# Attention transposes moved one step behind the scores, softmax sums sent through DRAM, and the ninth block put into the second half's PSUM bank

## The reference

```python
q_pool = q.reshape(B, H, S // 2, 2, D).mean(axis=3)          # S 1152, D 64: 576 queries a head
scores = scale * np.matmul(q_pool, k.transpose(0, 1, 3, 2))  # 576 x 1152 a head
scores = scores - np.max(scores, axis=-1, keepdims=True)
attn = np.exp(scores)
attn = attn / (np.sum(attn, axis=-1, keepdims=True) + 1e-09)
x = np.matmul(attn, v)          # -> 2304 tokens x 512
h = x @ w_in                    # 512 x 2048
g = np.maximum(h, 0.0) + alpha * np.minimum(h, 0.0)
return g @ w_out                # 2048 x 512
```

## Time and profile before

| | us |
|---|---|
| time, median of 3 runs (930.55 to 931.39) | 931.33 |
| the profiled execution, its own time | 932.26 |
| its span | 929.7 |
| PE busy in the span | 887.3 |
| DVE busy | 516.9 |
| ACT busy | 423.4 |
| POOL busy | 213.3 |

### The profile page before, as it was taken

The page is one execution under the profiler, slowest core; times in us unless marked ns, Lnnn a source line. Parts: engine busy times, 40 slices in busy tenths (PEclk is TensorE's granted clock), DMA queues, the critical chain, the costliest instruction groups (busy, mean ns, idle before and its releaser), DMA issues. The chain is left out here.

```text
span 929.7 us, 20770 instructions
## 1 busy us (share of the span) xinstructions
PE 887.3 (95%) x6896; PEld 623.2 (67%) x6896; DVE 516.9 (56%) x836; ACT 423.4 (46%) x963; POOL 213.3 (23%) x182
## 2 busy tenths in 40 slices
PE   3799999999999999999999999999999999999997
PEld 1455555555555555555545799989999999989995
DVE  2676767677767776767676344344444444343442
ACT  2566666666666666666666222222322222322222
POOL 2112111211121112111200323323232323323230
PEclk9999999999999999999999999999999999999999
DMA  7435423542354235523520122212422222322211
GB/s 186 106 83 135 119 65 82 133 121 63 82 133 123 60 82 133 127 57 82 133 71 1 59 68 58 67 62 63 136 57 68 57 68 61 132 59 66 65 36 68
DMA packets 36366, 79.57 MB, mean 86 GB/s; under 512 B 5360, under 2 KB 9456, under 8 KB 36336
## 3 DMA queue, kind: packets, MB, share of 16 engines
q1 hardware_dynamic: 33936, 74.48, 31.0%
q10 hardware_dynamic: 2400, 4.72, 1.5%
HBM read 74.46 MB, written 4.72 MB: 85 GB/s over the span
## 5 line engine op out<-in xcount | busy, mean ns | idle before, releaser
L432 DVE TENSOR_REDUCE neg_max<-s_ps 128x1 f32<-128x1152 f32 x144 | 194.1, 1348 | 16.6 <-DVEq L431 16.6
L573 PE MATMUL pv_ps<-pt,v_f 128*64 128x256 f32 (+1 forms) x1152 | 169.0, 414 | 0.0
L532 PE MATMUL s_ps<-k_f,q_f 64*128 64x512 f32 (+1 forms) x640 | 160.2, 626 | 5.2 <-PEq L543 5.2
L348 ACT ACTIVATE e_sb<-s_ps,neg_max 128x1024 f32<-128x1024 f32 x144 | 160.1, 1112 | 0.0
L587 PEld LDWEIGHTS slot_ps<-ident,e_sb 64*128 64x128 f32 x2304 | 86.0, 139 | 82.4 <-issue 82.4
L465 DVE COPY pt<-slot_ps 128x512 f32<-128x512 f32 x144 | 99.6, 692 | 61.3 <-DVEq L464 59.4
L341 ACT ACTIVATE e_sb<-s_ps,neg_max 128x128 f32<-128x128 f32 x144 | 52.9, 367 | 171.5 <-ACTq L340 171.5
L617 PE MATMUL slot_ps<-x_hi,wi_hi 128*128 128x384 f32 x384 | 129.5, 337 | 1.1 <-PEq L613 1.1
L617 PE MATMUL slot_ps<-x_lo,wi_hi 128*128 128x384 f32 x384 | 129.5, 337 | 0.0
L617 PE MATMUL slot_ps<-x_hi,wi_lo 128*128 128x384 f32 x384 | 129.0, 336 | 0.0
L479 DVE TENSOR_SCALAR e_sb<-slot_ps,alpha_sb 128x384 f32<-128x384 f32 x96 | 59.3, 618 | 123.2 <-DVEq L477 123.2
(11 more groups left out here) (46 smaller groups left out, 1098.8 us busy)
## 6 DMA issues: line engine op xcount, KB each, us to landing
q_raw<-in_q SPq DMA_DIRECT2D x64, 288.0 KB, 4.5
k_f<-in_k SPq DMA_DIRECT2D x64, 288.0 KB, 4.2
wi_raw<-in_w_in SPq DMA_DIRECT2D x48, 256.0 KB, 2.6
wo_raw<-in_w_out SPq DMA_DIRECT2D x48, 256.0 KB, 2.6
v_f<-in_v SPq DMA_DIRECT2D x32, 288.0 KB, 3.0
out<-pt ACTq DMA_DIRECT2D x6, 768.0 KB, 4.4
k_end<-in_k SPq DMA_DIRECT2D x64, 32.0 KB, 4.0
alpha_sb<-in_alpha SPq DMA_DIRECT2D x1, 8.0 KB, 4.7
```

Of the source, the lines that this page charges most:

```text
L348: nc.scalar.activation(e_sb[:, b * NKEY + at:b * NKEY + at + n], s_ps[:, S_AT[b] + at:S_AT[b] + at + n], ACT.Exp, bias=neg_max[:, b:b + 1] ...
L432: nc.vector.tensor_reduce(out=neg_max[:, b:b + 1], in_=s_ps[:, S_AT[b]:S_AT[b] + NKEY], op=ALU.max, axis=AX_X, negate=True).then_inc(max_r ...
L532: ins = nc.tensor.matmul(s_ps[to:to + m, S_AT[b] + at:S_AT[b] + at + BANK], q_f[2 * g + h][rows, first:first + m], k_f[2 * g + h][rows, at ...
L573: ins = nc.tensor.matmul(pv_ps[h * D:(h + 1) * D, 0:n], v_f[2 * g + h][:, a, :], pt[:, a, at:at + n], start=(a == 0), stop=(a == KT - 1))
```

## The change

1. **Lag.** In step `s`, PE now transposes tile `s - 1`. `e_sb` has three buffers instead of two. The wait for `exponential` of `s` moves from ahead of the transposes to ahead of `big_scores`. Everything that follows the transposes moves one step later (`PRODUCT`, `INVERT`, `SCALE`), and there is one more step at the end, which makes no scores.
2. **The ninth block.** It goes into the first 128 columns of `slot_ps[1]`, the bank that DVE empties. PE therefore waits for DVE's copy of that bank (`half1_copied`) ahead of the ninth transpose, and DVE waits for `ninth_ready` ahead of its copy of it. The score bank is no longer touched by it, and `bank2_ready` now tells of the small scores alone.
3. **Sums through DRAM.** `spread_inverse` and the ACT copy go. SP stores `inv_sum` (128 rows of 5 or of 4 values, transposed on the way) to a DRAM scratch `sums`, waits until that has landed, and loads it back twice, spread over 64 partitions each, into `inv_bc`. The store and the loads stand in SP's order between the other loads; the loads of `v` go behind them.
4. **Split of x.** `scale` writes the whole of `x` in fp32 (`x_f`). The two halves of pass 0 are split on POOL in the last steps of attention (`x_split`), those of passes 1 and 2 at the end of the pass before, by ACT (`x_high`, 1536 columns) and DVE (`x_low`, 1536 columns), and PE waits for `x_ready` ahead of the first `hidden_unit` of each half. The split parts of x, the weights and g lie in one tensor `ff`.

The core of the diff:

```diff
-    PRODUCT = {5: (0, (0, 1)), 6: (0, (2, 3)), 7: (0, (4, 5)), 8: (0, (6, 7, 8)),
-               0: (1, (0, 1)), 1: (1, (2, 3)), 2: (1, (4, 5)), 3: (1, (6, 7)), 4: (1, (8,))}
-    SPREAD = {6: 0, 1: 1}
-    INVERT = {4: 0, 8: 1}
-    FIRST = 6
+    PRODUCT = {6: (0, (0, 1)), 7: (0, (2, 3)), 8: (0, (4, 5)), 0: (0, (6, 7, 8)),
+               1: (1, (0, 1)), 2: (1, (2, 3)), 3: (1, (4, 5)), 4: (1, (6, 7)), 5: (1, (8,))}
+    INVERT = {5: 0, 0: 1}
+    SCALE = {1: 0, 6: 1}
+    FIRST = 7
...
-        NINTH = s_ps[:, 2 * BANK + P:2 * BANK + 2 * P]
+        NINTH = slot_ps[1][:, 0:P]
...
+            def store_sums(group):
+                a, b = GROUP_TILES[group]
+                sp.wait_ge(inv_ready, 1).then_inc(inv_ready, -1)
+                sp.dma_start(sums[a * P:b * P].rearrange("(t p) -> p t", p=P), inv_sum[:, a:b],
+                             allow_slow_non_contiguous=True).then_inc(inv_stored, 16)
+            def spread_sums(group):
+                _, _, n, first = GROUPS[group]
+                sp.wait_ge(inv_stored, 16).then_inc(inv_stored, -16)
+                for h in range(2):
+                    row = sums[GROUPS[group][h]:GROUPS[group][h] + n]
+                    sp.dma_start(inv_bc[h * D:(h + 1) * D, first:first + n],
+                                 row.rearrange("(o n) -> o n", o=1).to_broadcast([D, n])).then_inc(inv_bc_in[group], 16)
+            def sums_and_qk(pair, g):
+                store_sums(0)
+                load_q(pair * 2)
+                spread_sums(0)
+                sp.wait_ge(k_free[g], 1).then_inc(k_free[g], -1)
+                load_k(pair * 2, 2 * g), load_k(pair * 2 + 1, 2 * g + 1)
+                store_sums(1)
+                load_q(pair * 2 + 1)
+                spread_sums(1)
...
 PE, step:
-                pe.wait_ge(exp_done, 1).then_inc(exp_done, -1)
-                for i in range(2):
-                    pe.wait_ge(slot_free[i], 1).then_inc(slot_free[i], -1)
-                for a in range(2 * CH):
-                    at = s % 2 * NKEY + a * P
+                if s > 0:
                     for i in range(2):
+                        pe.wait_ge(slot_free[i], 1).then_inc(slot_free[i], -1)
+                    for a in range(2 * CH):
+                        at = (s - 1) % 3 * NKEY + a * P
...
+                if left >= 0:
+                    pe.wait_ge(exp_done, 1).then_inc(exp_done, -1)
                 if left > 1:
                     begin_scores(s + 2)
                     for ins in big_scores(s + 2):
                         ins.then_inc(s_ready, 1)
-                pe.wait_ge(ninth_free, 1).then_inc(ninth_free, -1)
+                if s > 0:
+                    pe.wait_ge(half1_copied, 1).then_inc(half1_copied, -1)
+                    transposed(s - 1, 2 * CH, NINTH).then_inc(ninth_ready, 1)
                 if left > 0:
                     pe.wait_ge(exp_cut_done, 1).then_inc(exp_cut_done, -1)
-                ins = transposed(s, 2 * CH, NINTH)
                 if left > 1:
-                    ins = small_scores(s + 2)
-                ins.then_inc(bank2_ready, 1)
+                    small_scores(s + 2).then_inc(bank2_ready, 1)
...
 DVE, step:
+                if t in SCALE and pair is not None:
+                    scale(SCALE[t], pair + (0 if s < 2 * TILES else 1))
+                    if SCALE[t] == 1:
+                        dve.sem_inc(v_free[1 - g], 1)
+                if s > 0:
+                    dve.wait_ge(tr_ready[1], 1).then_inc(tr_ready[1], -1)
+                    nc.vector.tensor_copy(pt_half((s - 1) % TILES, 1),
+                                          half_columns(slot_ps[1][:, :])).then_inc(half1_copied, 1)
...
+                if s > 0:
+                    dve.wait_ge(ninth_ready, 1).then_inc(ninth_ready, -1)
+                    nc.vector.tensor_copy(pt_ninth((s - 1) % TILES), NINTH).then_inc(slot_free[1], 1)
                 if left > 1:
+                    dve.wait_ge(bank2_ready, 1).then_inc(bank2_ready, -1)
                     row_max(s + 2)
```

More of the change, by code:

```diff
@@ L13, with build @@
 BANK = 512
-def build(nc, q, k, v, w_in, w_out, alpha, out):
+def build(nc, q, k, v, w_in, w_out, alpha, sums, out):
     HEADS, D, NKEY = k.shape
@@ L135, in build @@
         bank2_ready = sem("bank2_ready")
-        ninth_free = sem("ninth_free")
+        half1_copied = sem("half1_copied")
+        ninth_ready = sem("ninth_ready")
         slot_free = [sem(f"slot{i}_free") for i in range(2)]
         inv_ready = sem("inv_ready")
-        spread_ready = sem("spread_ready")
-        inv_bc_ready = sem("inv_bc_ready")
+        inv_stored = sem("inv_stored")
+        inv_bc_in = [sem(f"inv_bc{i}_in") for i in range(2)]
         pv_done = sem("pv_done")
         pv_free = sem("pv_free")
-        x_sb_free = sem("x_sb_free")
+        x_done = sem("x_done")
         x_hi_done = sem("x_hi_done")
@@ L178, in over_steps, with x_chunk, x_part @@
                     step(s, two * 2)
-            for s in range(FIRST, REST):
+            for s in range(FIRST, REST + 1):
                 step(s, 2 * BODIES, REST - 1 - s)
+        def x_chunk(n, h):
+            at = (2 * n + h) * TOK
+            return x_f[:, :].rearrange("p (d c) -> p d c", d=DT)[:, :, at:at + TOK]
+        def x_part(part, h):
+            return part[h].rearrange("p (d c) -> p d c", d=DT)
         def pt_half(t, half):
-            at = PT_AT[t] if half == 0 else PT_MIX if t == MIX else PT_AT[t] + HALF
+            at = PT_AT[t] + half * HALF
             return pt[:, 0:2 * CH, at:at + HALF]
@@ L403, in hidden @@
                     act.wait_ge(g_ready, 1).then_inc(g_ready, -1)
-                    nc.scalar.activation(g_hi[0][:, :], g_sb, ACT.Copy).then_inc(g_hi_done, 1)
+                    nc.scalar.activation(g_hi[0], g_sb, ACT.Copy).then_inc(g_hi_done, 1)
+                    if last and not last_pass:
+                        x_high(n + 1, 0)
                     if first:
@@ L414, in hidden @@
                     act.wait_ge(g_ready, 1).then_inc(g_ready, -1)
-                    nc.scalar.activation(g_hi[1][:, :], g_sb, ACT.Copy).then_inc(g_hi_done, 1)
+                    nc.scalar.activation(g_hi[1], g_sb, ACT.Copy).then_inc(g_hi_done, 1)
+                    if last and not last_pass:
+                        x_high(n + 1, 1)
                     if not (last_pass and isinstance(f, int) and f >= FT - 2):
@@ L443, in scale @@
                 dve.sem_inc(pv_free, 1)
-            def x_high(pair):
-                nc.vector.tensor_copy(x_hi[:, bass.ds(pair * NQ, NQ)], x_sb[:, :]).then_inc(x_hi_done, 1)
+                if group == 1:
+                    dve.sem_inc(x_done, 1)
             def invert(group):
@@ L501, in _, with x_low @@
             dve.wait_ge(alpha_in, 16).then_inc(alpha_in, -16)
[L502 to L503 removed]
+            scale(0, NPAIR - 1)
             for n in range(PASSES):
+                last_pass = n == PASSES - 1
+                def x_low(h):
+                    dve.wait_ge(x_hi_done, 1).then_inc(x_hi_done, -1)
+                    nc.vector.tensor_tensor(x_part(x_lo, h), x_chunk(n + 1, h), x_part(x_hi, h).bitcast(F32),
+                                            ALU.subtract).then_inc(x_ready, 1)
                 def hidden(f, i, first, last):
@@ L507, in hidden @@
                     if n == 0 and not first:
-                        scale(1)
-                        x_high(NPAIR - 1)
+                        scale(1, NPAIR - 1)
+                    if last and not last_pass:
+                        x_low(0)
                     unit(f, 1)
+                    if last and not last_pass:
+                        x_low(1)
                 over_hidden(dve, hidden)
@@ L545, in transposed @@
             def transposed(s, a, to):
[L546 removed]
+                at = s % 3 * NKEY + a * P
                 return nc.tensor.transpose(to, e_sb[:, at:at + P], ident[:, :])
[L549 to L562 removed]
             def product(group, g, tiles):
@@ L650, in _ @@
             over_steps(pe, step)
-            pe.wait_ge(x_ready, NPAIR - 2)
-            hidden_unit(0, 0, 0, 0)
+            hidden_unit(0, 0, 0, 0, 0)
             pe.wait_ge(slot_free[1], 1)
-            pe.wait_ge(ninth_free, 1).then_inc(ninth_free, -1)
-            product(1, 1, (0, 1))
-            spread_inverse(1, tail_ps)
-            product(1, 1, range(2, KT))
+            product(1, 1, range(KT))
             for n in range(PASSES):
```

201 lines of the change are left out of this document (83 added, 118 removed).

## The result

The changed kernel takes **969.89 us** (median of 4 runs, 966.65 to 971.02) against 931.12 (930.55 to 931.39) for the kernel before, timed beside it: a ratio of 1.041, 95% interval 1.039 to 1.044. The forecast was 936 with a range of 926 to 947. The sign was right and the size was not, by 34 us. The profiled execution is the quickest of the four, 966.65 with a span of 964.9 us.

The account below looks back on a forecast made before the run. PE was taken as the bound, its waits as what counts. Pairs + 2.1, start and end - 0.3, pass ends + 3.4, network start - 0.3 make + 4.9 on 932.26: 937.1, median 936.2, said as 936; range 926 to 947.

Parts of the forecast that it names:

- 15 pairs, undisturbed: Attention's 15 regular pairs: 31.05 us each against 30.91 before, + 2.1 us in all.
- start and end of attention: First steps and last steps of attention: together 32.3 us against 32.6 before, - 0.3 us.
- network: Splits of x at pass ends cost + 3.4 us; 8 spread matmuls fewer at the network's start give - 0.3.
- SP's queue: Store and load of the sums on SP take about 9 us, hidden with 8 us to spare.
- the sums come late: Rival: the sums' trip exceeds 17 us, each us beyond costing one in each pair; over 952 us, chance 0.06.
- the sum of a pair: One attention pair on PE: ninths 16.64, products 10.04 and smaller terms give 31.1 us, kept as 31.05, against 30.91.
- waits in a row: Rival: the small scores' own wait behind the ninth's adds 0.1 us in nine steps a pair; 941 to 952, chance 0.14.
- The whole new wait: PE's wait for DVE's copy ahead of the ninth transpose: ninths sum to 16.64 against 14.04, 2.6 us lost a pair.
- PE's own work: A pair in which PE never waits and spreads nothing takes 28.5 us, about 2.4 under today's 30.91.
- the two pass ends: Ends of network passes 0 and 1: splits of x make PE wait 1.7 us each, 3.4 in all.
- the last step: Step 144 at attention's end, with copies and weight splits behind its transposes: 3.8 us.

## Why the prediction was wrong

In the profiled execution the network's first matmul came 546.61 - 515.86 = 30.75 us later, and the network took 4.4 more. By the forecast's own terms:

| term | forecast | measured |
|---|---|---|
| 15 pairs, undisturbed | + 2.1 | + 14.2 (463.6 to 477.8, in the kernel without the trip) |
| 15 pairs, stalls | 0 | + 14.2 (477.8 to 492.0) |
| start and end of attention | - 0.3 | + 2.4 (start - 2.75, end + 5.1) |
| network | + 3.4 - 0.3 | + 4.4 (+ 3.4 in the kernel without the trip) |
| sum | + 4.9 | + 35.2 (span 929.7 to 964.9) |

**The failed step is the one on SP's queue**: "A small DMA takes 4.0 from issue to landing", "store and load, with issues, about 9", "Hidden, with 8 us to spare". The size of the trip was off and the kind of cost was missed. The store alone takes 8.2 to 11.5 us until its loads are issued, and the loads land some 4.3 after that (median of the larger ones). In the 15 pairs this is still hidden: DVE's scalings stand as far behind PE's product as in the kernel without the trip (0.29 or 0.95 us), in all cases but four, which are at most 0.22 later. Only the last trip of all isn't, the 12.8 us above, and costs 1.0 us in the network. What costs is what happens to others meanwhile. PE's announcements come up to 2.6 us late, PE stands 1.2 us inside its scores, and the loads of k land after 5.1 us instead of 4.2 (medians). Of the 14.2 us of stalls 3.7 are the lower clock behind the longest of them (PE is busy 448.5 us in the pairs, 444.8 without the trip).

The rival "the sums come late" named the store and priced another mechanism, a trip of over 17 us that the scaling waits for; in the changed kernel it came at the last trip alone, in a small form, and in a large one only with the store issued twice, where three scalings of the pairs stand 5 to 9 us behind PE's product. The price was taken from a load of k, of 32 KB in long rows; that row told neither the store's bytes (2.5 KB) nor its pieces. The page that was quoted there (the Trainium skill, DMA: Bandwidth & Descriptors, "Rules for kernel authors") has the rule that mattered, one descriptor for each element, and this case's trace agrees: 14,336 packets fewer in the one edit. The prediction named the rule, left its price open and thought only of the trip's length; the 2 us that it set beside it stand in a section on DMAs that GpSimd issues, and this store is SP's.

That the trip is the cause and not the order of the engines is shown three ways: by its removal (949.3), by its whole rows (950.1), and by its presence in a kernel that is otherwise the one before (968.5). By which path 512 or 640 small writes delay an announcement from PE to DVE stays open; nothing here separates the queue, the memory and the semaphores.

**The second failed step is the sum of a pair**, 31.05 against 31.85. The mechanism was right and two of its terms were small. The ninth stands at T + 1.73, not 1.70, in the ordinary step, 2.04 instead of 1.93 in step 1, and at 2.81 in step 6, as forecast. And the product follows it 0.54 behind, not 0.48, since the small scores have a wait of their own behind the ninth's. That was the rival "waits in a row", which priced it at 0.1 a step; swapped, the step has 0.45, so it is 0.09. Nine steps of 0.06 and the later ninths are 0.8 us a pair, 12 us in all. With 949.3 alone, this rival (941 to 952) would have held. The whole new wait is worth 2.86 us a pair (434.9 to 477.8), where the forecast took 2.6 from the ninths.

**What held.** The lag and the spread's absence win most of what was said, 30.91 to 28.94 a pair (28.5 forecast for PE's own work): 2.0 of 2.4. PE no longer waits ahead of the small transposes but 1.4 us in all. L538 took 1.76 (1.77 forecast), and the two pass ends delay PE by 2.1 and 1.7 us, together 3.8 (3.4). L538's value was a choice between 1.37 and 2.24, so that it came out is partly luck. Elsewhere in the network PE waits at its start, before the last unit as it did before (1.13, 1.12 before), and for the late last scaling. At the start the last step was longer than reckoned, 5.1 instead of 3.8: PE waits 1.32 ahead of the first unit, and 1.05 before.

## What to carry to other kernels

Before a transfer is called hidden, count its pieces, not only its bytes: 640 single values disturbed engines that never waited for them, and the same values in 128 pieces of 20 bytes, or turned by one 0.27 us transpose into 5 rows, disturbed nobody. A new wait on the engine that bounds the kernel costs in every step what it is late, and once more for each wait right behind it; put the one that is certain to be met first. When a change has two parts, one that wins and one that costs, try each alone: here the lag, with the sums off PE and the division left out, won 27 us (5 with the sums spread on PE as before, 17 with the sums turned) and was buried under the two others.
